# Soft mixture of experts on one core: second layer as eight 512-column products with partial sums per column tile, and token weights transposed from four copies made by GpSimd

## The reference, cut to what matters

```python
logits = x @ phi                              # 4608 x 32 slots
d = softmax over tokens (axis 0)              # 8 experts x 4 slots
slot_input = (d.T @ x).reshape(8, 4, 512)
for e in range(8):
    h = np.maximum(slot_input[e] @ w1[e], 0)  # 4 x 1024
    slot_out[e] = h @ w2[e]                   # 4 x 512
c = softmax over slots (axis 1)               # 4608 x 32
x = c @ slot_out
h = x @ w_in                                  # 512 -> 1024
...                                           # gate, layer norm, g_ln
return ln @ w_out                             # 1024 -> 512
```

## Time and profile before

| what | us |
|---|---|
| median of 3 runs | 485.13 |
| the three runs | 483.46 to 487.04 |
| the profiled execution, its own time | 483.38 |
| its span, first to last instruction | 481.5 |
| PE busy in the span | 442.7 |
| DVE busy | 320.5 |
| ACT busy | 254.3 |
| GpSimd busy | 248.4 |

### The profile page before, as it was taken

One profiled execution on the slowest core, in us unless ns is written; L12 is line 12 of the kernel. 1 busy time (PEld: TensorE's weight loads), 2 busy tenths in 40 slices (PEclk: granted clock), 3 DMA queues, 4 the chain that ended last, 5 costly groups with the idle time before them and its releaser, 6 DMA issues.

```text
span 481.5 us, 11183 instructions
## 1 busy us (share of the span) xinstructions
PE 442.7 (92%) x4125; PEld 359.9 (75%) x4125; DVE 320.5 (67%) x533; ACT 254.3 (53%) x550; POOL 248.4 (52%) x338
## 2 busy tenths in 40 slices
PE   1788999999999998888877999999999999999996
PEld 1668887888888885566755888887888888888885
DVE  7765777777777684633348797777777777777411
ACT  2355667586675844203227765555556655565310
POOL 0396787877878421000003333667666666666540
PEclk9998999999999999999997999999999999999999
DMA  8959697997979565999800026666666666666652
GB/s 274 290 147 307 223 273 258 326 222 286 318 247 271 191 242 183 360 399 395 308 3 1 22 50 126 135 130 134 129 133 134 135 134 135 134 133 133 135 123 48
DMA packets 125347, 91.79 MB, mean 191 GB/s; under 512 B 104824, under 2 KB 104832, under 8 KB 123264
## 3 DMA queue, kind: packets, MB, share of 16 engines
q1 hardware_dynamic: 125312, 91.32, 68.9%
HBM read 66.13 MB, written 9.44 MB: 157 GB/s over the span
## 4 chain that ended last, share of the span: by engine, by line
PE 76%; DVE 7%; SPq 7%; issue 4%; DMA 3%; ACT 3%; POOL 1%; DVEq 0%; ACTq 0%
PE banks L1431 11%; PE banks L1432 11%; PE banks L1430 11%; PE banks L1095 8%; SPq L432 6%; PE banks L1147 5%; PE banks L1083 4%; PE banks L1163 3%; PE banks L1311 3%; PE banks L1407 3%; PE banks L1331 3%; PE banks L1199 3%; PE banks L1127 2%; PE banks L1171 2%; PE banks L1347 2%
## 5 line engine op out<-in xcount | busy, mean ns | idle before, releaser
L1430 PE MATMUL banks<-wo_hi,uh 128*128 128x512 f32 x288 | 112.5, 391 | 0.0
L1431 PE MATMUL banks<-wo_lo,uh 128*128 128x512 f32 x288 | 112.1, 389 | 0.0
L1432 PE MATMUL banks<-wo_hi,ul 128*128 128x512 f32 x288 | 112.1, 389 | 0.0
L531 POOL TENSOR_TENSOR ul<-u_col,uh 128x1024 fp32r<-128x1024 f32 x30 | 72.2, 2406 | 32.1 <-ACT uh L560 32.1
L466 POOL TENSOR_TENSOR attn<-attn,srec 128x576 f32<-128x576 f32 (+1 forms) x40 | 45.9, 1148 | 61.5 <-DVE srec L813 61.5
L746 ACT ACTIVATE sq<-u,usum 128x1024 f32<-128x1024 f32 x36 | 41.5, 1153 | 42.0 <-DVE u L1016 42.0
L1430 PEld LDWEIGHTS banks<-wo_hi,uh 128*128 128x128 f32 x288 | 54.1, 188 | 11.2
L1432 PEld LDWEIGHTS banks<-wo_hi,ul 128*128 128x128 f32 x288 | 54.1, 188 | 11.3
L1431 PEld LDWEIGHTS banks<-wo_lo,uh 128*128 128x128 f32 x288 | 54.1, 188 | 11.1
L1006 DVE TENSOR_REDUCE nmax<-banks 128x1 f32<-128x1024 f32 x36 | 43.5, 1218 | 17.8 <-PE banks L1407 17.8
L1095 PE MATMUL banks<-kblk,qT 128*128 128x144 f32 (+1 forms) x320 | 50.8, 305 | 4.5 <-issue 2.4
(11 more groups left out here) (155 smaller groups left out, 751.3 us busy)
## 6 DMA issues: line engine op xcount, KB each, us to landing
wslot<-in_moe_w SPq DMA_DIRECT2D x14, 2048.0 KB, 10.1
u_col<-u_blk SPq DMA_DIRECT2D x240, 64.0 KB, 2.1
qb<-in_q SPq DMA_DIRECT2D x32, 256.0 KB, 6.3
out<-osb SPq DMA_DIRECT2D x32, 256.0 KB, 2.6
kraw<-in_k SPq DMA_DIRECT2D x8, 640.0 KB, 7.7
vraw<-in_v SPq DMA_DIRECT2D x8, 640.0 KB, 5.2
kraw<-in_k SPq DMA_DIRECT2D x8, 512.0 KB, 6.4
vraw<-in_v SPq DMA_DIRECT2D x8, 512.0 KB, 4.0
```

The source lines that it names most:

```text
L531: pool.tensor_tensor(ul[par][:, :, :].rearrange("p c (q t) -> p (c q) t", q=4), v, uh[par][:, :, :].bitcast(F32).rearrange("p c (q t) -> p ...
L1430: pe.matmul(ps[4 + par], uh[par][:, c, :], wo_hi[:, c, :], start=(c == 0), stop=False)
L1431: pe.matmul(ps[4 + par], uh[par][:, c, :], wo_lo[:, c, :], start=False, stop=False)
L1432: last = pe.matmul(ps[4 + par], ul[par][:, c, :], wo_hi[:, c, :], start=False, stop=(c == FC - 1))
```

## The change

Four things change. `so_t` makes eight products of 512 columns per expert instead of 32 of 128: chunk c goes to column tile c % 4, so the bank ends with four partial sums of all 512 output columns, on rows 32j to 32j+31. The sum over the four is made at the end: `so` becomes 128 by 512, copied in two halves, and four products with `fold4` (four identities of 32 by 32, one below the other) add the four row groups and transpose in one step. Third, GpSimd's `c_spread` copies each batch of c to four adjacent copies, and `c4_t(b)` is then five full transposes, of which the last, for the 64 short tokens, goes into ps[7]; group 8 is read from there after batch 7. Fourth, the waits: c4_t waits for the spread, the first also for gwc (ps[7] is in use until then), and the product with w_in waits for the last c4_lo in place of gwc.

```diff
-        so = bump("so", [P, P])
+        so = at("so", [P, DM], F32, attn_end + HALF)
         soT = bump("soT", [P, MC, SLOTS])
+        cs = [bump(f"cs{i}", [P, TILES, 4, SLOTS]) for i in range(2)]
...
+        def c4_bank(g):
+            return ps[5 + g % 2] if g < B else ps[7]
...
+            def c_spread(b):
+                if b >= 2:
+                    pool.wait_ge(sem("c4_ps"), b - 1)
+                pool.tensor_copy(cs[b % 2][:, :, :, :], c_all[:, b, :, :][:, :, None, :].to_broadcast([P, TILES, 4, SLOTS])).then_inc(sem("cs"), 1)
...
+            pool.wait_ge(sem("c_done"), 1)
+            for b in range(B):
+                c_spread(b)
...
             def c4_hi(g):
-                act.wait_ge(sem("c4_ps"), g + 1)
+                act.wait_ge(sem("c4_ps"), min(g + 1, B))
...
-            dve.tensor_copy(so[:, :], ps[3][:, 0:P]).then_inc(sem("so"), 1)
+            for n in range(2):
+                dve.tensor_copy(so[:, 256 * n:256 * (n + 1)], ps[3][:, 256 * n:256 * (n + 1)]).then_inc(sem("so"), 1)
...
                 for c in range(FC):
-                    for j in range(4):
-                        last = pe.matmul(ps[3][32 * j:32 * (j + 1), 0:P], hz[e % 2][:, c, :], w[:, c, P * j:P * (j + 1)],
-                                         start=(e == 0 and c == 0), stop=(e == E - 1 and c == FC - 1), tile_position=(0, 32 * j))
+                    j = c % 4
+                    last = pe.matmul(ps[3][32 * j:32 * (j + 1), :], hz[e % 2][:, c, :], w[:, c, :],
+                                     start=(e == 0 and c < 4), stop=(e == E - 1 and c >= 4), tile_position=(0, 32 * j))
...
-            def c4_t(g):
...
-                for n in range(4 if g < B else B):
-                    for j in range(4):
...
-                        last = pe.matmul(ps[5 + g % 2][32 * j:32 * (j + 1), o], i, r, start=True, stop=True, tile_position=(0, 32 * j))
+            def c4_t(b):
+                pe.wait_ge(sem("cs"), b + 1)
+                if b == 0:
+                    pe.wait_ge(sem("gwc"), FC)
+                if b >= 2:
+                    pe.wait_ge(sem("c4_lo"), b - 1)
+                for t in range(4):
+                    pe.transpose(c4_bank(b)[:, t * P:(t + 1) * P], cs[b % 2][:, t, :, :].rearrange("p a s -> p (a s)"), ident[:, :])
+                pe.transpose(ps[7][:, 64 * b:64 * (b + 1)], cs[b % 2][0:64, 4, :, :].rearrange("p a s -> p (a s)"), ident[0:64, 0:64]).then_inc(sem("c4_ps"), 1)
...
-            c4_t(8)
             so_t(7)
-            pe.wait_ge(sem("so"), 1)
-            pe.transpose(ps[4][:, 0:P], so[:, :], ident[:, :]).then_inc(sem("soT_ps"), 1)
+            for c in range(MC):
+                pe.wait_ge(sem("so"), c // 2 + 1)
+                last = pe.matmul(ps[4][:, c * SLOTS:(c + 1) * SLOTS], so[:, c * P:(c + 1) * P], fold4[:, :], start=True, stop=True)
+            last.then_inc(sem("soT_ps"), 1)
             pe.wait_ge(sem("soT"), 1)
-            pe.wait_ge(sem("gwc"), FC)
+            pe.wait_ge(sem("c4_lo"), C4_GROUPS)
```

More of the change, by code:

```diff
@@ L684, in c4_hi @@
             def c4_hi(g):
-                act.wait_ge(sem("c4_ps"), g + 1)
-                copy(c4[:, c4_cols(g)], ps[5 + g % 2][:, :]).then_inc(sem("c4_hi"), 1)
+                act.wait_ge(sem("c4_ps"), min(g + 1, B))
+                copy(c4[:, c4_cols(g)], c4_bank(g)[:, :]).then_inc(sem("c4_hi"), 1)
             def wo_high(n):
@@ L955, in c4_lo @@
                 o = c4[64:P, c4_cols(g)]
-                dve.tensor_tensor(o, ps[5 + g % 2][64:P, :], o.bitcast(F32), ALU.subtract).then_inc(sem("c4_lo"), 1)
+                dve.tensor_tensor(o, c4_bank(g)[64:P, :], o.bitcast(F32), ALU.subtract).then_inc(sem("c4_lo"), 1)
             def wo_low(n):
@@ L1329, in so_t @@
                 for c in range(FC):
-                    for j in range(4):
-                        last = pe.matmul(ps[3][32 * j:32 * (j + 1), 0:P], hz[e % 2][:, c, :], w[:, c, P * j:P * (j + 1)],
-                                         start=(e == 0 and c == 0), stop=(e == E - 1 and c == FC - 1), tile_position=(0, 32 * j))
+                    j = c % 4
+                    last = pe.matmul(ps[3][32 * j:32 * (j + 1), :], hz[e % 2][:, c, :], w[:, c, :],
+                                     start=(e == 0 and c < 4), stop=(e == E - 1 and c >= 4), tile_position=(0, 32 * j))
                 last.then_inc(sem("so_ps"), 1)
-            def c4_t(g):
[L1337 to L1340, removed]
-                for n in range(4 if g < B else B):
-                    for j in range(4):
[L1343 to L1346, removed]
-                        last = pe.matmul(ps[5 + g % 2][32 * j:32 * (j + 1), o], i, r, start=True, stop=True, tile_position=(0, 32 * j))
-                last.then_inc(sem("c4_ps"), 1)
+            def c4_t(b):
[7 more added lines that the diff above has]
+                pe.transpose(ps[7][:, 64 * b:64 * (b + 1)], cs[b % 2][0:64, 4, :, :].rearrange("p a s -> p (a s)"), ident[0:64, 0:64]).then_inc(sem("c4_ps"), 1)
             pe.wait_ge(sem("slotT_sb"), 1)
```

## The result

The changed kernel takes 478.09 us (median of 4 runs, 477.57 to 478.42) against 484.94 for the kernel before: a ratio of 0.9861, with a 95% interval of 0.9824 to 0.9897. In a second session it took 477.09 against 483.57, a ratio of 0.9857 (0.9827 to 0.9887). So it is faster by 1.4%, some 6.7 us; the forecast was 8.4 us and 476.7.

What follows compares the result with a forecast made beforehand. PE, starved of instruction packets beside the weight loads at 200 to 246 us, bounds the stage. The schedule moved w_in's product from 247.32 to 238.95, 8.4 us earlier, so 485.13 becomes 476.7 us (range 474.5 to 479).

Steps and rivals of the forecast that it cites:

- The gaps: PE's 1.0 to 1.3 us issue stops at 200 to 246 us: instruction packets come each 6.3 us; all go.
- The rival of gaps that stay: PE stops each 6.3 us whatever the instructions; gain only 4.2 us, 480.9 us; chance 0.13.
- the rule of the Trainium skill: Crossing into PE's next instruction block is mostly hidden; then fewer instructions remove no gaps and the gaps-stay sum holds, 480.9.
- so_t: Second-layer products on PE, 16 passes of 512 columns per expert: 1.86 us, no change (1.71 to 2.12).
- the rival of two tiles abreast: In so_t only two column tiles run at once: 3.72 us per expert, 489.7 us in all; chance 0.04.
- c_spread: GpSimd's eight copies of 128 by 640 elements: 1.4 us each (0.9 to 2.4), hidden.
- c4_t: Group of five transposes on PE: 0.6 us (0.5 to 0.7) instead of 1.01; c4_t(8), 1.1 us, is gone.
- The waits for hz and the tail: 1.9 us from c4_t(2) to so(5), 4.65 from c4_hi(6) to so's copy, then 1.92 to w_in's product.
- The floor: Last weights land at 229.3, 234.7 and 238.6 us whatever PE does; w_in's product may gain 8.7 us, no more.
- What follows moves along: Everything after w_in's product depends on m alone and shifts by the full 8.4 us.
- The rival of a longer half clock: More PE idling from 220 us brings another 1.2 GHz stretch, up to 3.4 us; gain 5.0, 480.1; chance 0.10.

Runs made afterwards that it cites:

- e3: Changed kernel with each product of 512 columns cut into four of 128 on the same column tile; 480.68 us, ratio 0.9922.
- e4: Kernel before without the six 2 MB weight loads for experts 5 to 7, which use weights of experts 0 to 2; 478.63 us, ratio 0.9869.
- e5: Changed kernel without the six 2 MB weight loads for experts 5 to 7; 476.20 us, ratio 0.9841.
- e6: Changed kernel with wo_low(3) on DVE moved behind the copy of soT; 474.16 us, ratio 0.9813.
- e10: Changed kernel with wo_low(3) moved behind soT's copy and hz of experts 5 to 7 ahead of c4_lo(2), (4), (6) on DVE; 477.30 us, ratio 0.9855.
- e2: Kernel before with only the spread and the full transposes of c4_t, second layer and tail as before; 480.36 us, ratio 0.9899.
- e12: Changed kernel with wo_low(3) moved behind soT's copy and identity transposes in PE's waits, 4 ahead of the fold; 472.84 us, ratio 0.9744.

## Why the prediction was right, and where it was off

*The gaps.* Right, and the larger part. The cause forecast from counting, more instructions than packets bring while the weights fill the DMA engines, is borne out by e3 (number up, gaps back, 6.33 us apart), by e4 (DMA quiet, gaps gone) and by the packets that land 1.2 to 1.5 us before each resumption. The rival of gaps that stay falls with both, and with it the sum worked out for the rule of the Trainium skill (page "Runtime: NRT & Kernel Launch", section "Instruction fetch mechanics") that such a crossing is mostly hidden: here it isn't, at 7.18 us in all. Of the gaps' price I had counted what the profile lists as idle; the schedule, made from starts, had it in full.

*so_t.* 1.86 us was taken, 1.83 measured. The column sums of the attention part were the right row, and the rival of two tiles abreast, at 3.72, falls.

*c_spread.* I took 1.4 us with 0.9 as the lower end; it took half of that:

```profile
L508 POOL COPY cs<-c_all x8: 716/721/723, 203.6 to 228.6; 128x640 f32<-128x640 f32 x8
```

The nearest rows were an addition with two inputs and a short cast, and neither gave the price of this copy. It was hidden either way: no engine waited for it.

*c4_t.* This is the mis-sized term. I took 0.6 us, from five transposes in a chain; behind so or hid a group takes 0.78 to 0.79 (214.99 to 215.77), and hT(4) with the group behind it 1.00 where I took 0.97. Four groups of the first kind lie on the path and come to some 0.75 us more, the two waits for hz to 0.1 more; so_t and the expert's period of 3.95 instead of 3.98 give 0.2 back. That is the difference of 0.70 between the forecast stage, 238.95 - 198.40 = 40.55 us, and the measured 41.25.

*The waits for hz and the tail.* Right. From the end of c4_t(2) to so(5) it took 1.96 us for 1.9; from c4_hi(6) to the copy of so 4.65 for 4.65; from there to the product with w_in 1.94 for 1.92. That DVE ends the stage and not w2's landing is shown by e5 and e6.

*The floor.* Half right. The loads did land as forecast (w2 of expert 7 at 216.5 + 19.1 = 235.6 in this profile, whose stage began 0.85 later), and e10 ran into them. I had added that "if PE's path is a microsecond shorter, nearly nothing is gained". The path that e6 shortened was DVE's, and it gained 0.80 us: w_in's last quarter landed at 237.2 there, 1.0 ahead of its product.

*"What follows moves along".* This step failed, by about 1 us: the stage gave 7.67 us and the medians differ by 6.5 to 6.9. In the profiles, from the product with w_in to the end of the span, before took 234.2 us, after 236.1, in the second profile 235.2. The first output tile is 0.5 us later both times, since the clock fell earlier: before, the first products with m still ran at full speed. The granted clock of the 23 us from that product on is 0.78 in both profiles, in before 0.85. The rival of a longer half clock was thus partly right, at 0.5 us and not 3.4. It isn't settled that the change brings it: e5, with the same order of work, had 0.93, and before has one profile. Another 1.4 us came later, most of it between output tiles 5 and 13. It was 0.5 in the second profile. SP's issue of the shuffles has 10% of the chain in both of these profiles and 6% in before (line 437 after, 432 before), so that share doesn't tell the two apart; I didn't test what sets it.

Together: forecast 8.4; the stage gave 7.7, the output stage took back some 1 us by the medians (1 to 2 in the profiles), and the medians differ by 6.5 to 6.9.

## What to carry to other kernels

Count PE's instructions per microsecond where the DMA engines are full of large loads: a matmul split into many narrow ones costs no PE time on column tiles, and yet 7 us here by the instructions it needs. When a stage gets shorter, look at what the engine at its end has queued that nobody needs yet (wo_low, 0.8 us), and at the granted clock behind it. A wait that replaces work can cost twice: once for itself, once for the products behind it at half clock, as in e10. Before a gain outside the changed stage is credited to an edit, compare the granted clock of the two profiles there: the first output tile moved by up to 1.6 us with it, between kernels with the same work at that place.

## What the runs showed of the hardware

A packet of 256 instructions came each 6.0 to 6.9 us beside a full stream of weights (before, e2, e3), whereas PE used one up in 5.1 us without a gap once the stream was off (e4). A packet travelled for 0.9 to 1.1 us beside the weights (before, e2, e3) and for 0.9 to 1.4 us without them (e4). What differs is how late it starts, by some 3 us of PE's work.

No single wait decides when the clock falls. It fell to 1.2 GHz around a wait of 1.66 us in e10, and was 1.00 across a stop of 2.13 us in e2. In e6 it was 0.57 of full from 193 to 197 us, after PE had waited 0.75, 0.47, 0.87 and 0.37 us; the changed kernel, with the same waits at the same place, kept 1.00 there (196 to 200 us).

34 cheap transposes kept it up over the turn to the output stage (e12), and the first output tile came 2.6 us earlier than in the changed kernel (21.05 and 23.62). That is more than the stretch's own products suggest: DVE and ACT, whose work waits for PE's, start earlier too. That last reason is argued from the order of the work and wasn't tested.
